# Scores of an attention scan as 64-row TensorE tiles, with R stored once and unpadded

## The reference, cut to what matters

```
for t in range(S):
    cur   = (u * k_t) outer v_t
    y_t   = r_t @ (state + cur)
    state = w_t[:, None] * state + k_t outer v_t
x = y as (B*S, H*D)
x = (sigmoid(x @ w_gate) * (x @ w_val)) @ w_out
out = elu(x @ w_in) @ w2_out
```

## Time and profile before

| | |
|---|---|
| median of 3 runs | 1202.37 us (1200.03 to 1205.33) |
| profiled execution, first to last instruction | 1203.3 us |
| TensorE busy | 1155.1 us, 96% |
| VectorE busy | 669.5 us, 56% |
| ScalarE busy | 472.2 us, 39% |
| GpSimd busy | 295.5 us, 25% |
| mean granted TensorE clock | 0.987 |

### The profile page before, as it was taken

How to read it: one execution, slowest core, us unless ns; L and a number is a source line. 1 busy time by engine, 2 the same in 40 slices (tenths; PEclk the granted TensorE clock), 3 DMA queues, 4 the chain that set the end, 5 groups by cost and what they waited for, 6 DMA issues and landing times.

```text
span 1203.3 us, 18133 instructions
## 1 busy us (share of the span) xinstructions
PE 1155.1 (96%) x6336; PEld 1006.2 (84%) x6336; DVE 669.5 (56%) x1044; ACT 472.2 (39%) x889; POOL 295.5 (25%) x290
## 2 busy tenths in 40 slices
PE   5778998999999999999999999999999999999999
PEld 4666777888888888888888888889999899899998
DVE  8777868494839393939393933354433334343433
ACT  2433444333333333333333333365544545454543
POOL 5563434143615351535153520000000000000000
PEclk9879998999999999999999999999999999999999
DMA  5451624122312231133204004220100101010000
GB/s 85 80 95 44 106 65 86 40 37 30 54 40 27 38 48 43 20 45 39 53 12 54 0 19 138 66 71 23 52 0 12 40 0 52 0 52 0 26 0 26
DMA packets 153413, 51.80 MB, mean 43 GB/s; under 512 B 126624, under 2 KB 148768, under 8 KB 153376
## 3 DMA queue, kind: packets, MB, share of 16 engines
q1 hardware_dynamic: 153376, 51.33, 21.0%
HBM read 41.88 MB, written 9.44 MB: 43 GB/s over the span
## 4 chain that ended last, share of the span: by engine, by line
PE 82%; DVE 11%; issue 4%; ACT 2%; DMA 0%; POOL 0%; DVEq 0%; SPq 0%; POOLq 0%; ACTq 0%
PE ps L606 21%; PE ps L639 17%; PE ps L631 16%; PE ps L615 10%; PE ps L544 7%; DVE RKW L828 6%; PE ps L560 3%; PE ps L534 3%; PE ps L565 2%; PE ps L573 2%; DVE hl L897 1%; DVE A L853 1%; DVE WS L917 1%; ACT RKW L669 1%; PE ps L581 1%
## 5 line engine op out<-in xcount | busy, mean ns | idle before, releaser
L606 PE MATMUL ps<-xh,WS 128*128 128x512 f32 x864 | 251.3, 408 | 1.6 <-DVE xl L888 1.6
L669 ACT ACTIVATE hh<-work 128x512 fp32r<-128x512 f32 x168 | 106.4, 633 | 287.5 <-DVE work L907 205.5
L544 PEld LDWEIGHTS ps<-RKW 128*128 128x128 f32 x1152 | 157.2, 203 | 59.1 <-DVE RKW L828 38.8
L544 PE MATMUL ps<-RKW 128*128 128x128 f32 x1152 | 167.6, 293 | 34.2 <-DVE RKW L828 34.0
L639 PE MATMUL ps<-WS,hh 128*128 128x384 f32 x768 | 198.0, 339 | 0.5 <-DVE hl L897 0.5
L828 DVE TENSOR_TENSOR RKW<-RKW,WL 64x256 f32<-64x256 f32 x288 | 186.1, 646 | 16.1 <-PE ps L544 13.7
L606 PEld LDWEIGHTS ps<-xh,WS 128*128 128x128 f32 x864 | 155.1, 190 | 30.7 <-issue 1.8
L897 DVE TENSOR_TENSOR hl<-work,hh 128x512 fp32r<-128x512 f32 x168 | 133.0, 791 | 85.3 <-ACT hh L669 84.3
L631 PE MATMUL ps<-xh,WS 128*128 128x512 f32 x576 | 164.2, 397 | 0.0
L615 PE MATMUL ps<-hh,WS 128*128 128x512 f32 x432 | 161.6, 411 | 0.4 <-DVE hl L897 0.3
L934 DVE SCALAR_TENSOR_TENSOR work<-work,ps 128x512 f32<-128x512 f32 x96 | 66.0, 688 | 172.2 <-ACT work L757 172.2
(11 more groups left out here) (67 smaller groups left out, 1324.7 us busy)
## 6 DMA issues: line engine op xcount, KB each, us to landing
nat<-in_w_dram SPq DMA_DIRECT2D x24, 192.0 KB, 3.7
nat<-in_k_dram SPq DMA_DIRECT2D x24, 192.0 KB, 4.8
nat<-in_r_dram SPq DMA_DIRECT2D x24, 192.0 KB, 5.2
V<-in_v_dram SPq DMA_DIRECT2D x24, 192.0 KB, 4.5
x_scratch<-work SPq DMA_DIRECT2D x6, 768.0 KB, 3.5
nat<-x_scratch SPq DMA_DIRECT2D x6, 768.0 KB, 5.2
out_dram<-Yt SPq DMA_DIRECT2D x5, 768.0 KB, 3.9
RKW<-in_moe_w_in_dram SPq DMA_DIRECT2D x16, 192.0 KB, 2.4
```

The costliest lines, as they stand in the source:

```text
L544: last = mm(bank[b][:, p * P:(p + 1) * P].rearrange("p (e i l) -> p e i l", e=2, l=L), K[:, g, :], Rb[:, :, :, 1, :], start=True, stop=True)
L606: last = mm(ps[:, VAL if val else GATE, :], gate_w(a, val, j, c), xp[b][:, c, :], start=(i == 0 and c == 0), stop=(i == 2 and c == KC - 1))
L669: return nc.scalar.activation(o, i, ACT.Copy)
```

## The change

A score product of a pair becomes two, one per head, on the rows of that head alone: 64 rows of K against 64 rows and 64 columns of R. Each head writes its own bank, so that a score part takes two banks, 4 x 64 columns in each, and two places in the rotation of three. R has the form of K, without zeros; the clearing of R falls, and so does `RP`: VectorE scales R in place for both heads in one instruction of 128 rows, also at L6, ScalarE evacuates R's transposes in one copy, and the last product of Y reads R. A is laid out head first, the masks are four times as long, and VectorE's and ScalarE's emptying reads both banks in one instruction.

```diff
-        RKW = sb("RKW", [P, 4 * G * P])
-        R = RKW[:, 0:2 * G * P].rearrange("p (g e t) -> p g e t", g=G, e=2)
+        RKW = sb("RKW", [P, 3 * G * P])
+        R = RKW[:, 0:G * P].rearrange("p (g t) -> p g t", g=G)
...
-        RP = W
-        A = sb("A", [P, G, 2, P])
+        A = sb("A", [P, 2, G, P])
...
+    SLOTS = []
+    for x in ORDER:
+        SLOTS += [x] * (2 if x[1][0] == "L" else 1)
...
+        def head_banks(hf, name, b):
+            at = SLOTS.index((hf, name, b))
+            return sorted((ATTN + at % NBK, ATTN + (at + 1) % NBK))
+        def scores(hf, name, b):
+            lo, hi = head_banks(hf, name, b)
+            return ps[:, lo:hi + 1:hi - lo, 0:PR * P // 2]
...
+            def bank_free(n, hf, name, i):
+                at = SLOTS.index((hf, name, i))
+                last = []
+                for m in range(at, at + (2 if name[0] == "L" else 1)):
+                    last.append(emptied(n if m >= NBK else n - 1, *SLOTS[m - NBK]))
+                if len(last) == 2 and last[0][0] is last[1][0]:
+                    last = last[1:]
+                for s, value in last:
+                    wait(pe, s, value)
...
                     for p, g in enumerate(pairs):
-                        Rb = R[:, g].rearrange("q e (i two l) -> q e i two l", two=2, l=L)
-                        last = mm(bank[b][:, p * P:(p + 1) * P].rearrange("p (e i l) -> p e i l", e=2, l=L),
-                                  K[:, g, :], Rb[:, :, :, 1, :], start=True, stop=True)
+                        for e in range(2):
+                            rows = slice(e * HP, (e + 1) * HP)
+                            Rb = R[rows, g].rearrange("q (i two l) -> q i two l", two=2, l=L)
+                            last = mm(ps[:, banks[e], p * HP:(p + 1) * HP].rearrange("p (i l) -> p i l", l=L),
+                                      K[rows, g, :], Rb[:, :, 1, :], start=True, stop=True)
...
-                    pe.wait_ge(a_rp, 2 * q + b + 1)
                     pe.wait_ge(d_r, level(q, NL - 1, b))
...
-                        last = mm(y[:, p].rearrange("p e d -> p (e d)"), RP[:, g, :],
+                        last = mm(y[:, p].rearrange("p e d -> p (e d)"), R[:, g, :],
...
-                    if x == 0:
-                        copy(R[0:HP, g, 0, :], src[0:HP])
-                        copy(R[HP:P, g, 1, :], src[HP:P]).then_inc(a_evac, 1)
-                    else:
-                        copy((None, K, W, KM)[x][:, g, :], src).then_inc(a_evac, 1)
+                    copy((R, K, W, KM)[x][:, g, :], src).then_inc(a_evac, 1)
...
-                        last = copy(A[s0:s0 + L, b * PR:(b + 1) * PR, :, s0 + L:s0 + 2 * L].rearrange("p g e t -> p (g e) t"),
-                                    src[s0:s0 + L, :, i, :])
+                        last = copy(A[s0:s0 + L, :, b * PR:(b + 1) * PR, s0 + L:s0 + 2 * L], src[s0:s0 + L, :, :, i, :])
                     last.then_inc(a_score, 1)
-                    if li == NL - 1:
-                        act.wait_ge(d_r, level(q, NL - 2, b))
-                        for e in range(2):
-                            rows = slice(e * HP, (e + 1) * HP)
-                            last = copy(RP[rows, b * PR:(b + 1) * PR, 0:L], R[rows, b * PR:(b + 1) * PR, e, 0:L])
-                        last.then_inc(a_rp, 1)
...
-                for e in range(2):
-                    rows = slice(e * HP, (e + 1) * HP)
-                    Rb = blocks(R[rows, pairs, e, :], L)[:, :, :, 1, :]
-
-                    out_R = blocks(RP[rows, pairs, :], L)[:, :, :, 1, :] if li == NL - 1 else Rb
-                    last = tt(out_R, Rb, Wb[rows, :, :, 0].to_broadcast([HP, PR, P // (2 * L), L]), ALU.mult)
-                last.then_inc(d_r, 1)
+                Rb = blocks(R[:, pairs], L)[:, :, :, 1, :]
+                tt(Rb, Rb, Wb[:, :, :, 0].to_broadcast([P, PR, P // (2 * L), L]), ALU.mult).then_inc(d_r, 1)
...
                         nc.vector.copy_predicated(
-                            blocks(A[:, pairs].rearrange("p g e t -> p (g e) t"), L)[:, :, :, 1, :],
-                            masks[:, li - 1, :].bitcast(I32).rearrange("p (i l) -> p i l", l=L).unsqueeze(1)
-                            .to_broadcast([P, 2 * PR, P // (2 * L), L]),
-                            bank[b].rearrange("p (x i l) -> p x i l", x=2 * PR, l=L)).then_inc(d_mask, 1)
+                            A[:, :, pairs].rearrange("p e g (i two l) -> p e (g i) two l", two=2, l=L)[:, :, :, 1, :],
+                            masks[:, li - 1, :].bitcast(I32).rearrange("p (x l) -> p x l", l=L).unsqueeze(1)
+                            .to_broadcast([P, 2, PR * P // (2 * L), L]),
+                            scores(hf, name, b).rearrange("p e (x l) -> p e x l", l=L)).then_inc(d_mask, 1)
...
-            nc.vector.memset(R, 0.0).then_inc(d_zero, 1)
```

More of the change, by code:

```diff
@@ L51, in build @@
     NBK = 3
-    assert ATT_BLK % NBK == 0
     EVAC = 8
@@ L66, in build @@
             [(0, "XT", i) for i in range(KC)]
-    AT = {use_of(*x): x for x in ORDER}
+    SLOTS = []
+    for x in ORDER:
+        SLOTS += [x] * (2 if x[1][0] == "L" else 1)
+    assert len(SLOTS) % NBK == 0
     GROUPS = []
@@ L143, in build @@
         hl = sb("hl", [P, 2, TOK], F32R)
-        masks = sb("masks", [P, NM - 1, P // 2])
+        masks = sb("masks", [P, NM - 1, PR * P // 2])
         ident = sb("ident", [P, P])
@@ L170, in build @@
                                                    ("a_evac", "a_sig", "a_hi", "a_xhi", "a_x2", "a_whi"))
-        a_score, a_rp = sem("a_score"), sem("a_rp")
+        a_score = sem("a_score")
         a_relu, a_exp, a_out = sem("a_relu"), sem("a_exp"), sem("a_out")
@@ L494, in _, with emptied @@
             mm = nc.tensor.matmul
[L496 to L503, removed]
+            def emptied(n, ph, pname, pi):
                 q = 2 * n + ph
                 if pname[0] == "T":
[L506 to L516, removed]
-                else:
-                    pe.wait_ge(d_xlo, KC * n + pi + 1)
+                    return a_evac, EVAC * q + 2 * STAGES.index(pname) + pi + 1
+                if pname == "KT":
+                    return a_evac, EVAC * q + 6 + pi + 1
+                if pname[0] == "L" and int(pname[1:]) >= NM:
+                    return a_score, level(q, int(pname[1:]) - NM, pi, NL - NM)
+                if pname[0] == "L":
+                    return d_mask, level(q, int(pname[1:]) - 1, pi, NM - 1)
+                if pname == "Y":
+                    return d_y, 2 * q + pi + 1
+                if pname == "S":
+                    return d_s, 4 * q + 2 * pi + 2
+                return d_xlo, KC * n + pi + 1
+            def bank_free(n, hf, name, i):
[7 more added lines that the diff above has]
+                    wait(pe, s, value)
             def attention(n, hf, name, b):
@@ L541, in attention @@
                     bank_free(n, hf, name, b)
+                    banks = head_banks(hf, name, b)
                     for p, g in enumerate(pairs):
-                        Rb = R[:, g].rearrange("q e (i two l) -> q e i two l", two=2, l=L)
-                        last = mm(bank[b][:, p * P:(p + 1) * P].rearrange("p (e i l) -> p e i l", e=2, l=L),
-                                  K[:, g, :], Rb[:, :, :, 1, :], start=True, stop=True)
+                        for e in range(2):
[3 more added lines that the diff above has]
+                                      K[rows, g, :], Rb[:, :, 1, :], start=True, stop=True)
                     last.then_inc(s_att, 1)
@@ L693, in attention @@
                     act.wait_ge(s_att, ATT_BLK * n + nth(hf, name, b))
-                    src = ps[:, attn_bank(hf, name, b), :].rearrange("p (x i l) -> p x i l", x=2 * PR, l=L)
+                    src = scores(hf, name, b).rearrange("p e (g i l) -> p e g i l", g=PR, l=L)
                     for i in range(P // (2 * L)):
                         s0 = 2 * L * i
-                        last = copy(A[s0:s0 + L, b * PR:(b + 1) * PR, :, s0 + L:s0 + 2 * L].rearrange("p g e t -> p (g e) t"),
-                                    src[s0:s0 + L, :, i, :])
+                        last = copy(A[s0:s0 + L, :, b * PR:(b + 1) * PR, s0 + L:s0 + 2 * L], src[s0:s0 + L, :, :, i, :])
                     last.then_inc(a_score, 1)
-                    if li == NL - 1:
-                        act.wait_ge(d_r, level(q, NL - 2, b))
-                        for e in range(2):
-                            rows = slice(e * HP, (e + 1) * HP)
-                            last = copy(RP[rows, b * PR:(b + 1) * PR, 0:L], R[rows, b * PR:(b + 1) * PR, e, 0:L])
-                        last.then_inc(a_rp, 1)
                 elif name == "XT":
```

25 lines of the change are left out of this document (11 added, 14 removed).

## The result

The changed kernel takes 1268.82 us (median of 4 runs, 1267.58 to 1269.57), the kernel before 1202.26 beside it: a ratio of 1.0548, 95% interval 1.053 to 1.0565. The profiled execution spans 1267.9 us against 1203.3, 64.6 more. The forecast was 1286, in a range of 1215 to 1375, slower.

What follows compares the result with a forecast made beforehand. TensorE was taken to bound the mixed blocks, an engine chain the stage alone. Banks and relief +35.5 (8 + 30 - 2.5) and switches +48 made +83.5 us: 1286 us, 8-in-10 range 1215 to 1375.

Steps and rivals of the forecast that it cites:

- The score part on TensorE: Each score part: 16 half loads side by side take 8 load times, 0.86 us, plus 0.5 us for array-mode switches.
- the right rival: The forecast itself, in each score part: halves load side by side and switches cost 0.5 us; chance 0.34.
- the 0.09 for an exposed load: At a switch: loads that can't run ahead add 0.09 us, beside 0.16 us of matmul tail.
- Banks in the mixed blocks: Mixed blocks: each score part waits until its predecessor is emptied; +3.0 us a half, +30 us over five blocks.
- the scaling's share: Bank waits on L1 to L3: VectorE's scaling of R taken at 0.65 us, plus 1.5 us a half behind GpSimd.
- the 0.4 put in for ScalarE: Mixed blocks: once per half ScalarE's copy of hh, waiting for VectorE, delays emptying; 0.4 us of waiting.
- The sum of a steady block: Steady mixed block: +6 us for banks and 0.5 us a part for switches in 24 parts, less added exit cover.
- First mixed block: First block mixing attention with layer 1: bank waits and switches as in the others, less 2.5 us for VectorE's relief.
- at most 5.2: First mixed block: VectorE's relief can give back at most 5.2 us; half was taken, -2.5 us.
- Stage alone: Attention of token block 0, running alone: nothing covers the bank waits; +3.8 us a half, +8 us.
- the 28.9 worked out: Stage alone, per half, first score part to first KT part: parts and their emptying in sequence, 28.9 us against 24.1.
- the clock as an open end: Stage alone: longer gaps could put more score parts at 1.2 GHz, 0.93 us each; not in the sum.

Runs made afterwards that it cites:

- the pair of runs: Changed kernel with one full 128-row product added to every score part: in its middle 1352.57 us, ahead of it 1307.22 us.
- The two runs with two scalings: Kernel before with only the change's bank rotation, 1301.7 us; changed kernel with R scaled by two 64-row instructions, 1332.48 us.
- filled kernel before: Kernel before with four added 128x128 products behind each score part where attention runs alone: 1209.19 us, ratio 1.0042.
- bank waits alone: Kernel before with only the change's bank rotation, each score part taking two places but writing one bank: 1301.7 us.

## Why the prediction was near, point by point

*The score part on TensorE.* Right: the parts are bound by loads, the halves load side by side, and 16 half loads take the 0.97 us that 8 full ones took. The chosen value, the switch cost on top of it, was the right rival, mis-sized: 0.5 a part put in, 0.31 measured by the pair of runs, 0.35 by the chain against parts of the kernel before whose loads ran ahead. The entry costs 0.10 (0.33 from the last 512-column matmul to the first of the part, against 0.235), because the load starts some 0.07 before the tail is over and the matmul starts with it; the 0.09 for an exposed load was not to be added. With the drain that the Trainium skill states (TensorEngine Tiling (Array Packing), Key Properties) the trace agrees: loads no longer run ahead over a switch, and the first starts 0.07 before the recorded end of the last matmul.

*Banks in the mixed blocks.* Mechanism right, size wrong: 3.5 us a half put in, 0.24 to 0.5 measured. On L1 TensorE waits 0.24 and 0.25, after that nowhere. The step that failed is the scaling's share. I took 0.65 and added 1.5 a half for GpSimd's long products; VectorE's merged scaling starts first and takes 0.43, on average over the steady blocks too, and it is GpSimd's scaling of K beside it that is longer (its mean rose from 771 to 867 ns). With 0.12 + 0.43 + 1.31 = 1.86 against a cover that the exit made 1.60, L1 should wait 0.26, as it does, and L2 and L3 not at all; nor did the 0.4 put in for ScalarE show. The two runs with two scalings show that the waits of the prediction and more, 10 to 14 us a block, are there as soon as that instruction is doubled.

*The sum of a steady block.* 24 x 0.31 = 7.4, + 0.8 for banks, - 1.1 of old waiting gives 7.1, and the blocks got longer by 7.0 to 7.2 us apart from the gaps at the turn of the loop (0.38 to 0.91 us). Forecast: 15.6.

*First mixed block.* The step "at most 5.2" failed, and by its reading: the stretch 94.1 to 221.1 ends at a mark inside the block, so that it misses 9 us of it. The whole block had 14.2 us over a steady one, with VectorE at 101.3. The change took 21.7 us off VectorE, and the excess is 3.9. Forecast +13, measured -2.6. That VectorE's relief did this is argued from these rows; no run isolates it.

*Stage alone.* Forecast +8, measured +36.5, the largest miss. The order of parts is as described, and the waits too: 12 parts and their emptying from 14.69 to 52.33, 37.6 us against the 28.9 worked out. The 8.7 are the 12 parts at 1.97 in place of 1.15 (9.8), less a little on the scalings. Over both halves the score parts are 25 of the 36.5; the other 11 are Y, S and the transposes at the lower level, 3.28 for Y where it had been 1.72. The prediction named the clock as an open end and gave 0.93 a part as its price, but left it out of the sum, and it had no price for the stages that are not score parts. This is the step that failed: 24 x 0.93 = 22 more would have left some 6 us of the miss. Why the clock fell is open. What the runs show is a price of 32 us for the banks as they were rotated here, at a clock that stays low with them or without.

*The total.* Of the forecast's 83.5 us, the switches were 11 too high (48 against 120 x 0.31 = 37), the banks in the mixed blocks 31 (30 against 5 x (0.8 - 1.1) = -1.5) and the relief of the first block 7 too small (2.5 against 7.1 + 2.6 = 9.7). The stage alone was 28 too low, and 2 us of gaps at the turn of the loop were not in it. 83.5 - 11 - 31 - 7 + 28 + 2 = 64.5, with 64.6 measured. That the sum came within 17 us is luck, errors of both signs and not four good terms.

## What to carry to other kernels

Half-array tiles that alternate save load time only against twice as many full loads; set beside the padded full-array product they replace, they bring nothing when loads bind, as here, and each island of them among full-array matmuls costs two switches. When a buffer's rotation is tightened, price the whole chain from the part's end to the release, in the engine's own order: here one instruction in front of the releasing one, 0.4 us long and 0.9 where another engine's held it, was worth 10 us a block, on an engine that had been all but covered before. And compare stages between the same two marks.

## What the runs showed of the hardware

A switch from products of 128 rows to products of 64 and back costs 0.31 us in blocks where TensorE is busy 140.5 of 141.6 us. Loads of 128 f32 columns follow each other after 0.111 us with 128 rows, 0.085 with 64 rows on the same half, 0.052 on alternating halves. TensorE was busy without a gap for 29.7 us on products of 64 columns at a granted clock of 0.50, 1.2 GHz, all that time; in the stage alone of the filled kernel before, busy 70.5 of 82.0 us on products of 128 columns, it was 0.98. The gaps of 0.4 to 0.9 us at the turn of the loop appear in the ten kernels where the page counts 49 and more packets of instructions on its queue q8, and not in the two with 20, before and bank waits alone; the body of the loop of the filled kernel before is unchanged, so its place in the program or what runs ahead of it matters. Which, no run tells.
